# A later pair's exponentials ahead of the rounding copy in the first stage of a three-part transformer kernel, with tables and weight splits moved early

## The reference

```
# 1: windowed attention, 8 heads of 64, window 128, with a distance bias
scores = q @ k.T / 8 - slope[h] * |i - j|      # masked unless 0 <= i - j < 128
x = softmax(scores) @ v                        # heads side by side: [576, 512]
# 2: gated MLP with mixing over positions
h = relu(x @ w_in);  u, v = halves of h        # 512 columns each
v_n = (v - mean(v)) / sqrt(var(v) + 1e-6)
x = (u * (w_spatial @ v_n + b_spatial)) @ w_out
# 3: four causal attention experts, two of them chosen for each position
out = sum over the top 2 experts of w_e * (softmax(q_e @ k_e.T / 8) @ v_e @ wo_e)
```

## Time and profile before

| | us |
|---|---|
| time, 3 runs | 641.71, 641.88, 642.42 (median 641.88) |
| the profiled execution | 642.28 |
| its span, first to last instruction | 640.4 |
| busy in it: PE, DVE, ACT, POOL | 581.9, 363.5, 331.3, 264.4 |
| mean granted clock of TensorE | 0.966 of full speed |

### The profile page before, as it was taken

How to read it: one execution, slowest core, us unless ns; L and a number is a source line. 1 busy time by engine, 2 the same in 40 slices (tenths; PEclk the granted TensorE clock), 3 DMA queues, 4 the chain that set the end, 5 groups by cost and what they waited for, 6 DMA issues and landing times.

```text
span 640.4 us, 13316 instructions
## 1 busy us (share of the span) xinstructions
PE 581.9 (91%) x4456; PEld 496.9 (78%) x4456; DVE 363.5 (57%) x1239; ACT 331.3 (52%) x971; POOL 264.4 (41%) x453
## 2 busy tenths in 40 slices
PE   3897979997999999997998999998899999999796
PEld 1576978696876779996876678998786788999684
DVE  4787442255668763245665874236566884226663
ACT  2777422244658754243656774234565874234563
POOL 5567233024644443334553353351573453341431
PEclk9899989997999999998998999999799999999798
DMA  8804512000000050020001014020010000000011
GB/s 239 231 2 95 153 65 75 0 1 1 35 15 29 2 131 20 1 75 2 33 10 38 3 43 107 1 75 2 0 42 35 2 3 2 1 0 1 2 38 39
DMA packets 29757, 26.37 MB, mean 41 GB/s; under 512 B 5811, under 2 KB 22195, under 8 KB 29685
## 3 DMA queue, kind: packets, MB, share of 16 engines
q1 hardware_dynamic: 29684, 25.46, 14.0%
HBM read 20.74 MB, written 4.72 MB: 40 GB/s over the span
## 4 chain that ended last, share of the span: by engine, by line
PE 65%; DVE 13%; issue 7%; POOL 6%; ACT 5%; DMA 1%; SPq 1%; POOLq 0%; DVEq 0%; ACTq 0%
PE bank L1070 15%; PE bank L1072 14%; PE bank L1071 14%; PE bank L1096 7%; PE bank L1060 6%; POOL p L517 3%; PE bank L1081 3%; PE bank L1242 2%; PE bank L1243 2%; DVE pt_lo L834 2%; DVE ring L772 2%; ACT pt_hi L587 1%; ACT x_hi L592 1%; ACT ring L562 1%; DVE neg L918 1%
## 5 line engine op out<-in xcount | busy, mean ns | idle before, releaser
L1070 PE MATMUL bank<-pt_hi,vv 128*64 128x128 f32 (+1 forms) x528 | 106.6, 233 | 11.9 <-DVE x_lo L841 7.1
L430 POOL TENSOR_SCALAR ring<-ring,r 128x256 f32<-128x256 f32 (+2 forms) x160 | 72.0, 462 | 105.8 <-DVE r L784 105.5
L834 DVE TENSOR_TENSOR pt_lo<-bank,pt_hi 128x512 fp32r<-128x512 f32 (+5 forms) x176 | 84.2, 494 | 44.7 <-ACT pt_hi L587 43.1
L587 ACT CAST pt_hi<-bank 128x512 fp32r<-128x512 f32 (+5 forms) x176 | 72.8, 433 | 68.9 <-PE bank L1096 64.8
L1071 PE MATMUL bank<-pt_lo,vv 128*64 128x128 f32 (+1 forms) x528 | 102.2, 225 | 0.0
L1072 PE MATMUL bank<-pt_hi,vv 128*64 128x128 f32 (+1 forms) x528 | 102.2, 225 | 0.0
L517 POOL TENSOR_SCALAR p<-p,r,wgt 128x128 f32<-128x128 f32 (+4 forms) x80 | 51.6, 648 | 114.2 <-DVE r L784 57.0
L1070 PEld LDWEIGHTS bank<-pt_hi,vv 128*64 128x64 f32 x528 | 72.8, 138 | 25.2 <-issue 21.2
L562 ACT ACTIVATE ring<-ring,neg 128x256 f32<-128x256 f32 (+2 forms) x160 | 75.1, 473 | 20.4 <-DVE neg L772 20.4
L1060 PE MATMUL bank<-kz,q 128*128 128x512 f32 (+2 forms) x160 | 74.8, 560 | 11.9 <-DMA kz<-kT 9.2
L1071 PEld LDWEIGHTS bank<-pt_lo,vv 128*64 128x64 f32 x528 | 72.9, 138 | 7.8 <-issue 1.7
(11 more groups left out here) (132 smaller groups left out, 1545.8 us busy)
## 6 DMA issues: line engine op xcount, KB each, us to landing
q<-qT SPq DMA_DIRECT2D x16, 256.0 KB, 3.7
kz<-kT SPq DMA_DIRECT2D x32, 128.0 KB, 3.9
v_raw<-v SPq DMA_DIRECT2D x16, 256.0 KB, 4.1
out<-o_sb SPq DMA_DIRECT2D x16, 256.0 KB, 2.0
w_in_raw<-w_in SPq DMA_DIRECT2D x2, 1024.0 KB, 7.1
w_cat_raw<-wcat SPq DMA_DIRECT2D x1, 1544.0 KB, 6.7
w_spatial_raw<-wsT SPq DMA_DIRECT2D x1, 1152.0 KB, 11.9
w_outT_raw<-woT SPq DMA_DIRECT2D x1, 1024.0 KB, 5.1
```

The source lines that it names most:

```text
L430: last = nc.gpsimd.tensor_scalar(p, p, r1[0:r, i % 2, h:h + 1], 0.0, ALU.mult, ALU.add)
L587: last = nc.scalar.copy(pt_hi[0:r, g % 2, c0:c1], bank[0:r, 2 + g % 2, c0:c1])
L834: last = nc.vector.tensor_tensor(pt_lo[0:r, g % 2, c0:c1], bank[0:r, 2 + g % 2, c0:c1], pt_hi[0:r, g % 2, c0:c1].bitcast(F32), ALU.subtract)
L1070: nc.tensor.matmul(to, hi_l, hi_r, start=first, stop=False)
```

## The change

The diff has four parts.

1. ACT: in iteration g of stage 1, in all batches, `exp1(g+3)` moves from behind `high_pt(g)` and `high_x` to the head of the iteration.
2. DVE: `reciprocal1(g+3)` moves from behind `bias1(g+4)` to the head of the iteration, and the second `low_x` half moves from before `low_pt(g)` to behind it.
3. POOL, batch 0: the tables move to the program's head, ahead of the first splits of `v`, and no longer wait for four scaled groups.
4. Batch 0: `w_spatial` is rounded on ACT in iterations 13 to 17 of stage 1. The rests of its four full tiles move from DVE to POOL (iterations 13 to 16, ahead of a `v` split where there is one). The last tile with its bias row stays on DVE, now between `norm_v` of the last block but one and `stats_v` of the last. A semaphore `s_wsl` counts the four on POOL.

```diff
-            def tables():
-
-                pool.wait_ge(s_tab, 1)
-                pool.wait_ge(s1_sd, AHEAD1)
-                nc.gpsimd.memset(ws_raw[LAST:P, NT - 1, :], 0.0).then_inc(s_wz, 1)
...
+            pool.wait_ge(s_tab, 1)
+            nc.gpsimd.memset(ws_raw[LAST:P, NT - 1, :], 0.0).then_inc(s_wz, 1)
...
+                def low_w_spatial(t):
+                    pool.wait_ge(s_whi, 2 * KT + t + 1)
+                    nc.gpsimd.tensor_tensor(ws_lo[:, t, :], ws_raw[:, t, :], ws_hi[:, t, :].bitcast(F32), ALU.subtract
+                                            ).then_inc(s_wsl, 1)
+
                 for g in range(NG1):
                     if g + AHEAD1 - 1 < NG1:
                         scale1(b, g + AHEAD1 - 1)
-                    if first and g == 0:
-                        tables()
+                    if first and 13 <= g < 13 + NT - 1:
+                        low_w_spatial(g - 13)
...
                 for g in range(NG1):
+                    if g + AHEAD1 - 1 < NG1:
+                        exp1(b, g + AHEAD1 - 1)
                     for qb in range(NT - 1):
                         if g == END1[qb] + 2:
                             high_x(qb, 1)
...
                     for qb in range(NT - 1):
                         if g == END1[qb] + 2:
                             high_x(qb, 0)
-                    if g + AHEAD1 - 1 < NG1:
-                        exp1(b, g + AHEAD1 - 1)
...
+                    if first and 13 <= g < 13 + NT:
+                        high_w_spatial(g - 13)
...
                 for g in range(NG1):
+                    if g + AHEAD1 - 1 < NG1:
+                        reciprocal1(b, g + AHEAD1 - 1)
                     for qb in range(NT - 1):
                         if g == END1[qb] + 2:
                             low_x(qb, 1)
+                    low_pt(g, G1, ORDER1, s1_h, s1_l, keys1(ORDER1[G1[g][0]]))
+                    for qb in range(NT - 1):
                         if g == END1[qb] + 2:
                             low_x(qb, 0)
-                    low_pt(g, G1, ORDER1, s1_h, s1_l, keys1(ORDER1[G1[g][0]]))
                     if g + AHEAD1 < NG1:
                         bias1(b, g + AHEAD1)
-                    if g + AHEAD1 - 1 < NG1:
-                        reciprocal1(b, g + AHEAD1 - 1)
...
+                norm_v(NT - 2)
                 if first:
-                    for t in range(NT - 1):
-                        low_w_spatial(t)
-                norm_v(NT - 2)
+                    low_w_spatial_last()
                 stats_v(NT - 1)
                 norm_v(NT - 1)
-                if first:
-                    low_w_spatial(NT - 1)
...
-                            pe.wait_ge(s_wlo, 2 * KT + NT + 1)
+                            pe.wait_ge(s_wsl, NT - 1)
+                            pe.wait_ge(s_wlo, 2 * KT + 2)
```

More of the change, by code:

```diff
@@ L234, in build @@
         s_whi, s_wlo = sem("weights_hi"), sem("weights_lo")
+        s_wsl = sem("w_spatial_lo")
         s_base, s_bt, s_wz = sem("bias_base_ready"), sem("bias_table_chain"), sem("w_spatial_border_zero")
@@ L385, in _ @@
                                     pattern=[[-1, P]], channel_multiplier=1).then_inc(s_tab, 1)
-            def tables():
-                pool.wait_ge(s_tab, 1)
-                pool.wait_ge(s1_sd, AHEAD1)
-                nc.gpsimd.memset(ws_raw[LAST:P, NT - 1, :], 0.0).then_inc(s_wz, 1)
[L392 to L406, removed]
+            pool.wait_ge(s_tab, 1)
+            nc.gpsimd.memset(ws_raw[LAST:P, NT - 1, :], 0.0).then_inc(s_wz, 1)
+            pool.wait_ge(s_wz, 1)
+            link(nc.gpsimd.tensor_copy(identr[:], ident[:]))
+            link(nc.gpsimd.memset(causal[:], 0.0))
+            link(nc.gpsimd.affine_select(out=causal[:], in_=causal[:], compare_op=ALU.is_ge, fill=MASKED, base=0,
+                                         pattern=[[-1, P]], channel_multiplier=1))
+            link(nc.gpsimd.tensor_copy(causalr[:], causal[:]))
+            link(nc.gpsimd.memset(neghalf[:], -0.5))
+            link(nc.gpsimd.memset(logits[:], 0.0))
+            link(nc.gpsimd.memset(brow[:], 1.0))
+            link(nc.gpsimd.memset(brow[LAST:LAST + 1], 0.0))
+            link(nc.gpsimd.memset(before[:], 0.0))
+            for e in range(1, E):
+                link(nc.gpsimd.memset(before[:, e, 0:e], 1.0))
+            nc.gpsimd.memset(rank[:], 0.0).then_inc(s_tab, 1)
             def split_v_hi(b, t):
@@ L639, in row @@
                 high_x(NT - 1, 0)
-                if first:
-                    for t in range(NT - 1):
-                        high_w_spatial(t)
                 relu_u(3)
@@ L648, in row @@
                 high_vn(NT - 1)
-                if first:
-                    high_w_spatial(NT - 1)
                 relu_u(6)
@@ L806, in low_w_in, with low_w_spatial_last @@
                                         ).then_inc(s_wlo, 1)
[L808 to L814, removed]
+            def low_w_spatial_last():
+                t = NT - 1
+                dve.wait_ge(s_whi, 2 * KT + NT)
+                nc.vector.tensor_tensor(ws_lo[0:LAST, t, :], ws_raw[0:LAST, t, :], ws_hi[0:LAST, t, :].bitcast(F32),
+                                        ALU.subtract).then_inc(s_wlo, 1)
                 dve.wait_ge(s_tab, 2)
@@ L1267, in out_product @@
                     if i == 0 and first:
-                        pe.wait_ge(s_wlo, 2 * KT + NT + 2)
+                        pe.wait_ge(s_wlo, 2 * KT + 3)
                     for k in range(2):
```

## The result

| | before | after |
|---|---|---|
| time, median (4 runs each, side by side) | 641.8 | 673.79 (672.75 to 675.76) |
| ratio to before | | 1.052, 95% interval 1.047 to 1.056 |
| the profiled execution, its span | 642.28, 640.4 | 673.55, 671.7 |
| busy: PE, DVE, ACT, POOL | 581.9, 363.5, 331.3, 264.4 | 590.0, 365.7, 334.1, 269.1 |
| mean granted clock | 0.966 | 0.962 |

The account below looks back on a forecast made before the run. PE was taken to set stage 1's pace before the change, a series through ACT and DVE after it. 26.6 + 1.5 - 0.3 = 27.8 us on 642.28 gave 670 us; own range 662 to 677, 8-in-10 range 652 to 682.

Parts of the forecast that it names:

- The pace: Stage 1, iterations 0 to 3: ACT and DVE hops in series take 2.36 us a turn, against PE's 1.63.
- Batches 1 to 3: Stage 1: batches 1 and 3 lose 9.3 us each, batch 2 loses 8.0; 26.6 us, plus 1.5 for the clock.
- one loop: Stage 1, from one high_pt to the next: pt_hi, pt_lo, first bias and two exponentials all run in series.
- Rival A: Stage 1: PE keeps its pace, the series is hidden and only stalls go; 628 us, chance 0.03.
- Batch 0: Whole batch: 0.8 us lost up to values1(4), 3.1 to values1(16), 4.2 gained at its end; -0.3 in sum.
- a late split of `v`: POOL, batch 0: three subtractions ahead of the last v split delay values1(16) by 0 to 4.4 us, taken as 0.5.
- a hold-up of `vn`: Batch 0: each of POOL's four subtractions could hold up a DVE instruction by up to 1.45 us, 5.8 in all.
- The end of batch 0: Last w_spatial chain: the 3.28 us stall and the half clock behind it go, 0.7 stays; gain 4.2 us.
- The clock: Stage 1, behind new stalls of about 2.4 us: mostly covered slower PE, 0.5 us for each of three batches.
- rival C: Stage 1: each 2.4 us stall lowers the clock with PE uncovered, eight times 1.6 us; 681 us, chance 0.10.
- Rival B: Stage 1: only the first five iterations cost, extra items later find slack; 652.5 us, chance 0.12.
- D: Whole kernel: the loop costs just what batch 0 gives back, 8.5 us; near 642 us, chance 0.02.

Follow-up runs that it names:

- kernel 5: The changed kernel with bias1(g+4) moved ahead of low_pt(g) on VectorE: 664.17 us, ratio 1.038 to the kernel before.
- kernel 2: The kernel before with only stage 1's new order on ScalarE and VectorE, without the moved work: 674.86 us, ratio 1.051.
- kernel 1: The changed kernel with stage 1's old order on ScalarE and VectorE, moved tables and w_spatial work kept: 640.11 us, ratio 0.997.
- kernel 6: The changed kernel with stage 1's old order, moves kept, and GpSimd's four w_spatial subtractions behind iterations 16 to 18: 636.23 us, ratio 0.992.

## Why the prediction came out right, and what in it was wrong

The forecast was 670 us and 673.8 were measured, inside both ranges. By the spans, 31.3 us were lost where 27.8 were forecast.

- **The pace.** Right. 2.36 us were forecast for iterations 0 to 3, 2.31 measured, by the hops that were added up.
- **Batches 1 to 3.** Right in the main. Up to V4 of batch 1, 5.1 us later was forecast and 5.1 measured (213.19 less 204.75, less the 3.4 us that batch 0 had left). From V4 to V16, 4.2 was forecast and 4.9 came. Batch 2 lost 3.1 and 5.8 (3.8 and 4.2 forecast), batch 3 4.6 and 5.8. That is 29.3, and the rest of batch 3 was 1.4 shorter, so 27.9; forecast with the clock 28.1. That the two are so close is luck in part: up to V4 1.2 less came than forecast, from V4 to V16 2.4 more with the clock counted in.
- **What the terms stood for.** Partly wrong. The steps had `x_hi` behind the exponentials in their sums, so the total held; but the text put it all down to one loop, and the loop is 9.6 us of 33.7. Rival A's condition was read too narrowly for the same reason: a loop shorter than PE's pace is not enough, as kernel 5 shows with 1.7 us and 664 us.
- **Batch 0.** The term that was wrong: -0.3 forecast, +3.4 measured. 0.8 of that is the start of the first scores, at 10.02 us in place of 9.23. Twelve kernels with the new head began them between 9.25 and 10.32, 9.65 on average, and the two with the old head at 9.23 and 9.37, so most of it is spread. From there to V4 0.8 was lost, as forecast. From V4 to V16, 35.9 was forecast and 39.55 came. Up to V12 it is 1.8 more than in batch 1 (26.24 against 24.41), where 1.2 had been set down for two `w_in_lo`. V12 to V16 took 13.31, and in kernel 2, which has the new order but not the moved work, 10.85. Most of these 2.5 us is the clock, for which the forecast had no term here. The `pt_hi` that follows the second transposes behind V12, ACT of the changed kernel and of kernel 2:

```profile
63.68 0.59 ACT L590 CAST pt_hi<-bank 128x512 fp32r<-128x512 f32 x1 [1.16 <-PE bank L1092]
```

```profile
61.29 0.57 ACT L587 CAST pt_hi<-bank 128x512 fp32r<-128x512 f32 x1
```

  It comes 6.40 us after V12 in place of 4.77, and it waited for PE, which was busy all the time at a clock of 0.50 and reached those transposes 5.74 us after V12 in place of 3.28. That is 1.6 of the 2.5 us. 0.8 is left for the moved work, which the forecast had at 0.5, but for another reason, a late split of `v`. What the rows show is a longer `vn` (0.54 in kernel 2) and a `w_spatial_hi` of 0.67 us ahead of `x_hi` on ACT, which the forecast had put at nothing. It had named a hold-up of `vn` in words, but without a term:

```profile
65.46 1.17 DVE L855 TENSOR_SCALAR vn<-v_sb,mv,rstd 128x512 f32<-128x512 f32 x1
```

  The same moved work costs far more in the old order: V12 to V16 is 14.77 us in kernel 1 where it was 10.65.
- **The end of batch 0.** The 3.28 us stall is 0.66 now, and the spatial product takes 15.9 us from its first start to its last, not 17.4, at full clock: 5.0 gained, 4.2 forecast.
- **The clock and rival C.** C's mechanism came true at seven of eight stalls; its price of 1.6 us each holds only where nothing covers PE. Batches 2 and 1 of the changed kernel have the same instructions and the same stall before V12, with the clock at 0.59 and 1.00 behind it. PE reached the second transposes behind V12 after 4.89 and 3.29 us, 1.6 apart, but V16 after 11.19 and 10.46, 0.7 apart: the rest was covered while ACT's turns led, as the forecast said. Its 0.5 us for each of three batches was a little low, and batch 0 lost 1.6. Where the loop is cut, the whole price shows. Kernel 5 waited 2.05 us before V4 in batch 2 and 2.03 in batch 1:

```profile
364.40:368.40 4.00, 3.96 (x16) 2.73 (x17) 1.95 (x9) 1.05 (x4) 0.93 (x2) 0.57 0.00 0
209.40:213.40 4.00, 4.00 (x25) 2.82 (x26) 2.59 (x12) 2.05 (x8) 0.94 (x3) 1.00 0.00 0
```

  V4 to V8 took 12.00 us at the lower clock and 10.39 at the full one. The forecast read from the kernel before that stalls of 2.37 and 3.28 us were followed by a lower clock and one of 1.34 was not. It left out one in between, 2.06 us before V12 of batch 0 (PE at 51.55), with full clock behind it:

```profile
51.50:55.50 4.00, 3.95 (x38) 3.51 (x39) 3.82 (x15) 2.92 (x12) 2.12 (x4) 1.00 0.00 0
```

- **Rival B** (the early iterations only) fell: V4 to V16 lost 5 to 7 us a batch. A and D fell with the time.

## What to carry to other kernels

Moving work that is needed later ahead of work that is needed now, in in-order queues, costs twice: it can close a loop over the engines (add up the hops of one turn and compare with the bound engine's pace), and it puts its own length and its own waits ahead of what the bound engine is about to need. A loop that is short enough is not yet an order that is good: look at the places where something else must pass, as a block change. Idle time on a second engine is no free room if its instructions hold up the one you wait for, as GpSimd's did VectorE's `vn` here: put its long instructions where nothing of the other is urgent (3 to 4 us in kernel 6).
